# Third tile's Fourier features before the first transposes, VectorE's sums first in each pair, low parts of the up weights a pair ahead

## The reference, cut to what matters

```python
def _attn_ref(q, k, v, lam):          # 2 batches, 8 heads, 768 tokens, 64 wide
    for b in range(nb):               # blocks of 64 tokens
        intra = (qb @ kb.T * Dmask) @ vb
        out[block] = intra + (qb * lam_pow) @ kv_state
        kv_state = lam_block * kv_state + (kb * rev_pow).T @ vb

def _moe_ref(x, w_ch1, w_ch2):        # x is 2 x 768 x 512
    X = np.fft.fft(np.fft.fft(x, axis=1), axis=2)
    u = x + np.real(X)
    un = (u - mean(u)) / sqrt(var(u) + 1e-6)
    return u + np.maximum(un @ w_ch1, 0.0) @ w_ch2      # 512 -> 2048 -> 512

def _moe2_ref(x, g_ln, w_ch1, w_ch2): # the same without the transform, with a gain g_ln
    ...
```

## Time and profile before

| | |
|---|---|
| median of 3 runs | 627.78 us (626.17 to 630.95) |
| the profiled execution | 626.12 us |
| its span, first to last instruction | 624.2 us |
| mean granted TensorE clock | 0.981 |
| busy: TensorE, VectorE, ScalarE, GpSimd | 595.3, 371.4, 242.6, 151.9 us |

### The profile page before, as it was taken

The page is one execution under the profiler, slowest core; times in us unless marked ns, Lnnn a source line. Parts: engine busy times, 40 slices in busy tenths (PEclk is TensorE's granted clock), DMA queues, the critical chain, the costliest instruction groups (busy, mean ns, idle before and its releaser), DMA issues.

```text
span 624.2 us, 10828 instructions
## 1 busy us (share of the span) xinstructions
PE 595.3 (95%) x4124; PEld 409.2 (66%) x4124; DVE 371.4 (60%) x637; ACT 242.6 (39%) x488; POOL 151.9 (24%) x133
## 2 busy tenths in 40 slices
PE   6999799978989999999999999999999999999997
PEld 3999656745666666666666666576666666666664
DVE  2468967968678586556676898733345334433223
ACT  0223133653465432443356675234422344232231
POOL 1536664643532000110322763001000010000000
PEclk8699799989999999999999999999999999999999
DMA  7999790000000253231122231100001000010001
GB/s 227 330 372 390 275 316 9 1 2 0 1 2 1 71 166 103 102 101 43 60 68 86 85 119 51 35 2 1 1 28 42 1 2 0 1 68 1 1 2 68
DMA packets 41412, 50.43 MB, mean 81 GB/s; under 512 B 2442, under 2 KB 28690, under 8 KB 39956
## 3 DMA queue, kind: packets, MB, share of 16 engines
q1 hardware_dynamic: 39156, 45.05, 22.0%
q10 hardware_dynamic: 1728, 3.15, 1.3%
q0 software_dynamic: 480, 1.57, 0.9%
HBM read 43.46 MB, written 6.30 MB: 80 GB/s over the span
## 4 chain that ended last, share of the span: by engine, by line
PE 70%; DVE 13%; issue 7%; POOL 5%; ACT 3%; DMA 2%; SPq 0%; DVEq 0%; ACTq 0%; POOLq 0%
PE bank L572 30%; PE bank L552 26%; PE bank L472 4%; PE bank L409 3%; PE bank L404 2%; PE bank L374 2%; DVE arena L1034 1%; DVE arena L1042 1%; DVE arena L1155 1%; DVE arena L1035 1%; PE bank L541 1%; POOL arena L1410 1%; DVE arena L1149 1%; PE bank L387 1%; DVE arena L1163 1%
## 5 line engine op out<-in xcount | busy, mean ns | idle before, releaser
L572 PE MATMUL bank<-arena 128*128 128x512 f16 x1152 | 287.0, 379 | 3.0 <-DVE arena L1163 2.1
L552 PE MATMUL bank<-arena 128*128 128x256 f16 x2016 | 261.4, 274 | 9.7 <-DVE arena L1204 6.7
L552 PEld LDWEIGHTS bank<-arena 128*128 128x128 f16 x2016 | 197.6, 98 | 84.5 <-DVE arena L1204 7.6
L572 PEld LDWEIGHTS bank<-arena 128*128 128x128 f16 x1152 | 112.3, 98 | 89.6 <-DVE arena L1163 2.7
L1155 DVE SCALAR_TENSOR_TENSOR arena<-arena 128x512 f16<-128x512 f32 x96 | 71.4, 744 | 75.7 <-ACT arena L804 75.6
L804 ACT ACTIVATE arena<-arena 128x512 f16<-128x512 f32 x96 | 60.4, 629 | 101.3 <-DVE arena L1204 95.9
L1198 DVE SCALAR_TENSOR_TENSOR arena<-bank,arena 128x256 f32<-128x256 f32 x48 | 20.2, 421 | 70.9 <-PE bank L552 70.9
L1367 POOL TENSOR_TENSOR arena<-arena 128x512 f32<-128x512 f32 x6 | 8.5, 1412 | 150.8 <-ACT arena L775 90.8
L1149 DVE TENSOR_TENSOR arena<-arena 128x512 f16<-128x512 f32 x42 | 36.3, 873 | 12.2 <-ACT arena L788 12.2
L859 ACT ACTIVATE arena<-bank 128x256 f32<-128x256 f32 x48 | 18.4, 383 | 58.4 <-PE bank L552 58.4
L968 DVE TENSOR_REDUCE arena<-arena 128x1 f32<-128x1024 f32 x32 | 38.3, 1208 | 0.0
(11 more groups left out here) (97 smaller groups left out, 553.0 us busy)
## 6 DMA issues: line engine op xcount, KB each, us to landing
arena<-w SPq DMA_DIRECT2D x48, 256.0 KB, 4.5
arena<-w SPq DMA_DIRECT2D x24, 512.0 KB, 3.7
arena<-attn SPq DMA_DIRECT2D x10, 1024.0 KB, 8.3
x_dram<-arena ACTq DMA_DIRECT2D x12, 256.0 KB, 6.3
out<-arena SPq DMA_DIRECT2D x12, 256.0 KB, 2.1
arena<-attn SPq DMA_DIRECT2D x4, 512.0 KB, 4.3
arena<-c SPq DMA_DIRECT2D x1, 1153.5 KB, 11.1
arena<-g SPq DMA_DIRECT2D x1, 514.0 KB, 12.5
```

Source lines behind the costliest of these rows:

```text
L552: last = nc.tensor.matmul(bank_, wst[:, i, wx, w, kt, :], xs[s % 2][:, ux, x, kt, :], start=not started and k == 0, stop=k == 5, skip_grou ...
L572: last = nc.tensor.matmul(ops[t][:], hT[n % 2][:, half, hx, t * P:(t + 1) * P], wdn[:, i, wx, half * DM:(half + 1) * DM], start=first and ...
```

## The change

It moves instructions and adds no work. The sets of instructions on all engines are the same.

- TensorE: `features(2)` runs ahead of the first transposes, right behind `sequence(12)`; `sequence(13)` runs behind them. The last of the four transposes of stage 0 goes to bank 2 in place of bank 4, and so the transposes wait for `y_done` 12, and sequences 14 and 15 for the copies of the transposes (`ev_done` 4).
- ScalarE's prelude: `up_hi(0,1)` ahead of the first `q_rows`, `q_rows(2)` ahead of `turned`, `down_hi(0,0)` earlier, `y_columns(13)` to `(15)` each a step later.
- VectorE's prelude: `walls(1,2)` and `power_of_two(1)` between `combine(0)` and `combine(1)`; `combine(2)` ahead of the `x_lo`, `down_lo(0,0)` between the second and the third of them.
- VectorE's pairs: `up_lo(0, i+2)` in pair i behind the sums z21 and z22 and the first `hidden_lo`; before it was `up_lo(0, i+1)` ahead of the sums. `row_scale` in the third pair of every stage moves behind the sums as well.
- GpSimd: `up_sums(0,1)` ahead of `add_rows(0)`; `add_rows(2)` between `x_sum(0,1)` and `x_sum(0,2)`.

```diff
--- before.py
+++ after.py
@@ -185,7 +185,7 @@
         kvps = [bank[6 + b] for b in range(B)]
         f1_bank = bank[0:3]
         chain, seventh, spare, ops = [bank[0][:, 0:HT], bank[1][:, 0:HT]], bank[2], bank[3], bank[4:8]
-        first_turn = [bank[3], bank[6], bank[7], bank[4]]
+        first_turn = [bank[3], bank[6], bank[7], bank[2]]
 
         pow_dram = nc.dram_tensor("pow_dram", [H, PITCH], F32).ap()
         x_dram = nc.dram_tensor("x_dram", [B * S, DM], F32).ap()
@@ -650,14 +650,16 @@
             spread_back(1, 2)
             middle_row(0)
             features(1)
-            sequence(range(F1_FIRST, 14))
+            sequence(range(F1_FIRST, 13))
+            features(2)
             pe.wait_ge(fix_done, 1)
             pe.wait_ge(wall_done, 2)
+            pe.wait_ge(y_done, 12)
             for k in range(KT):
                 turn(0, k)
+            sequence(range(13, 14))
+            pe.wait_ge(ev_done, NT)
             sequence(range(14, 16))
-            pe.wait_ge(ev_done, NT)
-            features(2)
 
             for n in range(PAIR * STAGES):
                 pair(n)
@@ -871,27 +873,27 @@
             act.wait_ge(x_out[1], 16 * NBLK)
             up_hi(0, 0)
             y_columns(8)
+            up_hi(0, 1)
             q_rows(0)
             q_rows(1)
             for f in range(9, 12):
                 y_columns(f)
             deviation(0)
-            up_hi(0, 1)
             y_columns(12)
-            y_columns(13)
+            q_rows(2)
             for k in range(KT):
                 turned(0, k)
             x_hi(0, 0)
             x_hi(0, 1)
-            y_columns(14)
+            down_hi(0, 0)
+            y_columns(13)
             x_hi(0, 2)
             x_hi(0, 3)
-            y_columns(15)
+            y_columns(14)
             x_hi(0, 4)
             x_hi(0, 5)
-            down_hi(0, 0)
+            y_columns(15)
             x_hi(0, 6)
-            q_rows(2)
             for n in range(PAIR * STAGES):
                 pair(n)
 
@@ -1187,12 +1189,8 @@
                     combine(LATE[n])
                 if n == 2 * PAIR:
                     tops(2, 5)
-                if prep is not None and i == 2:
-                    row_scale(prep)
                 if prep is not None and i >= 5:
                     x_lo(prep, 2 * i - 9)
-                if s == 0 and 1 <= i < SLOTS - 1:
-                    up_lo(0, i + 1)
                 dve.wait_ge(p4_done, n + 1)
                 dve.wait_ge(u2_out, n + 1)
                 nc.vector.scalar_tensor_tensor(z[n % 2][:, 1, 0:HT], seventh[:, 0:HT], H_SCALE, u2, ALU.mult,
@@ -1207,7 +1205,11 @@
                 if s > 0 and i == 0:
                     add_residual(s - 1, 0)
                     add_residual(s - 1, 1)
+                if s == 0 and i < SLOTS - 2:
+                    up_lo(0, i + 2)
                 if prep is not None:
+                    if i == 2:
+                        row_scale(prep)
                     if n > 0 and i == 0:
                         statistics(prep, (0, 1))
                     if n == 1:
@@ -1261,19 +1263,20 @@
             up_lo(0, 0)
             tops(1, 2)
             combine(0)
+            walls(1, 2)
+            power_of_two(1)
             combine(1)
             statistics(0, range(NT))
-            walls(1, 2)
             row_scale(0)
             normalise(0, range(NT))
-            power_of_two(1)
+            up_lo(0, 1)
+            combine(2)
+            x_lo(0, 0)
+            x_lo(0, 1)
+            down_lo(0, 0)
+            for k in range(2, 7):
+                x_lo(0, k)
             out_scale(0)
-            up_lo(0, 1)
-            for k in range(6):
-                x_lo(0, k)
-            down_lo(0, 0)
-            x_lo(0, 6)
-            combine(2)
             dve.wait_ge(osc_done, 1)
             for n in range(PAIR * STAGES):
                 if n == PAIR * GROUPS:
@@ -1410,13 +1413,15 @@
                     last = nc.gpsimd.tensor_tensor(u, u, mirror(DE[j % 2][:, half, :], half), ALU.add)
                 last.then_inc(addA, 1)
 
+            up_sums(0, 1)
             add_rows(0)
             add_rows(1)
-            up_sums(0, 1)
-            for k in range(4):
-                x_sum(0, k)
+            x_sum(0, 0)
+            x_sum(0, 1)
+            add_rows(2)
+            x_sum(0, 2)
+            x_sum(0, 3)
             up_sums(0, 2)
-            add_rows(2)
             add_rows(3)
             up_sums(0, 3)
             add_rows(4)
```

## The result

| | before | changed |
|---|---|---|
| median of 20 runs each | 626.69 us (625.19 to 631.13) | 629.75 us (627.75 to 631.24) |
| profiled execution, span | 626.12, 624.2 us | 629.07, 627.1 us |
| mean granted TensorE clock | 0.981 | 0.977 |
| TensorE busy | 595.3 us | 597.0 us |

The ratio is 1.0043, with a 95% interval of 1.0029 to 1.0056: 3.1 us more by the medians, 2.9 by the spans. That is within the 1% called no change in advance, but with 20 runs of each the interval lies wholly on the slow side.

A forecast was written before the change was run, and what follows sets the result against it. TensorE bounds the steady pairs; only 110 to 200 us and a 0.3 us wait in stage 2 can move the end. 1.85 plus 1.0 gives 2.85 us more, on a 627.8 us median: 630.6 us, range 624 to 634.5.

The forecast's parts named there:

- d(6): First down group of pair 6 on TensorE, forecast at 197.4 us, 1.85 us behind the kernel before.
- 1.0 in stage 2: row_scale behind the sums delays normalise; stage 2's transposes wait 1.3 us instead of 0.3, 1.0 behind; bounds 0 to 2.
- d(1): First down group of pair 1 on TensorE, forecast at 133.25 us, a gain of 2.0, bounds 0.8 to 4.0.
- signs of being right: Included TensorE idle 3 to 5 us ahead of pair 0 and 1 to 2 us before its last product.
- By turns on the ports: Ahead of pair 0, VectorE and GpSimd alternate instruction by instruction on SBUF; pair 0 begins at 122.3 instead of 118.1.
- the second rival: New waits for y_columns(15) and down_lo put TensorE's clock down: 7.1 us more, 634.9 us; chance 0.1.
- d(2): First down group of pair 2, forecast at 146.95 us, 0.15 ahead of before, after late_features wait 2.1 us.
- d(3): First down group of pair 3, forecast at 161.1 us, 0.1 ahead of before, after waiting 2.3 us for down_lo(0,2).
- the 4.7: TensorE's old waits of 2.4, 1.6 and 0.7 us behind pair 0, up to pair 4, all forecast to go.
- d(4): First down group of pair 4, forecast at 176.4 us, 1.6 behind before, after waiting 3.1 us for down_lo(0,3).
- the waits simply go: Rival for pairs 0 to 5: slack keeps the gains, 7.7 us less, 620.1, chance 0.1; half kept, 624.3, chance 0.15.
- The clock as the way to the slow side: Rival: TensorE's clock falls at new waits ahead of pair 0 and behind down_lo; 7.1 us more, 634.9 us, chance 0.1.

The follow-up runs named there:

- the third experiment: Changed kernel with up_lo(0, i+2) moved to the end of its pair, behind down_lo, the second hidden_lo and normalise: 626.28 us, ratio 0.9974 to the kernel before.
- the second experiment: Kernel before with the pairs of the changed kernel, its own prelude untouched: 632.25 us, ratio 1.0076.
- the last: Changed kernel with up_lo(0,4) alone moved, from pair 2 to pair 3 behind combine(5): 630.01 us, ratio 1.0054 to the kernel before.
- the first four experiments: New prelude with old pairs, 624.52 us; old prelude with new pairs, 632.25; changed kernel with up_lo at pair's end, 626.28, or with GpSimd's weight sums earlier, 623.93.
- the fastest kernel: Changed kernel with weight sums and y_columns(15) earlier, row_scale behind the sums only in stage 0, up_lo placed pair by pair: 618.36 us, ratio 0.9865.

## Why the prediction was right, and which steps were not

It forecast 2.85 us more; 2.9 by the spans and 3.1 by the medians came. (The 630.6 us forecast stood on three runs of the kernel before, 627.78; with 20 runs its median is 626.69, and the changed kernel came at 629.75.) Both parts of the sum were right too: 1.85 behind at d(6) (2.4 measured) and 1.0 in stage 2 (0.8 measured, and 0.9 undone by its experiment).

**Pair 0.** The gain was to be 2.0, with d(1) at 133.25; it came at 132.82, a gain of 2.3. The reason given is confirmed: VectorE's last sum releases the last product (forecast to end at 130.5, measured 130.1), and that product runs at full clock. Several steps were off. The wait ahead of it was to be 1.7 us and is 0.52; the stretch ahead of pair 0 was to be 3 to 5 us and is 2.84. Both lie outside what was named as signs of being right. By turns on the ports, `x_sum(0,2)` was to end at 121.0 and pair 0 to begin at 122.3 after 3.9 us; ScalarE's split of its result starts at 120.00 and pair 0 begins at 121.13 after 2.84. I had the two engines taking turns at every instruction, and they lost less than that. And the clock fell at this wait, which the forecast gave to the second rival. Wait and fall together cost 0.8 us at d(1), by the experiment with `y_columns` one place earlier, which took both away: the path over `features(3)`, the copy of Q and `combine(3)` was not in the forecast, which had VectorE bound by its own list alone. How the 0.8 us divide between the wait and the fall was not tried.

**Pairs 1 and 2.** Late_features were to wait 2.1 us and d(2) to come at 146.95: 2.17 and 146.85. For d(3) a wait of 2.3 and 161.1: 2.22 and 161.35. The waits for the sums in these pairs are gone, as said. One count in the forecast does not hold together: it lets the wait of 1.6 us in pair 4 go, among the 4.7, and two items further on keeps 1.2 of it. It belonged to ScalarE's copy behind `up_hi(0,5)` and not to a sum that the change serves earlier.

**The transposes of stage 1** are the step that was wrong. They were to start at 162.65, waiting for nothing new. They started at 163.90, and what they wait for is the second difference of `combine(5)`, which ends at 163.80. I had read their line as waiting for `normalise` and overlooked the second semaphore. Here the semaphore itself costs only the wait of 0.31 us. Of the 1.25 us by which the transposes are late, 0.25 is d(3) and some 0.7 the clock, which was down after d(3) (six matmuls in 1.48 at 162.11). It stayed without effect: the delays went into slack ahead of d(4), where the wait shrank from the 3.1 I forecast to 2.29. d(4) came at 176.40 where 176.4 was forecast, because it is set by VectorE and GpSimd, not by TensorE. That the two agree so closely is partly luck: `up_hi(0,5)` came 0.2 us late, and the `x_sum` beside `up_lo(0,5)` cost 1.0 us instead of 1.35. For the same reason the 1.2 us at the second product of pair 4 did not show: TensorE was itself late. In the third experiment, where `down_lo` is no longer in the way, the same semaphore costs 3.2 us and brings a fall of the clock of 2.9, and there it spoiled the expectation.

**The port.** The forecast needed an `x_sum` that makes `up_lo(0,5)` wait: L1036 takes 2.29 us at 171.92 beside it. `up_hi(0,5)` came at 168.71 for 168.5. The Trainium skill ("SBUF — State Buffer", section Who interferes with whom) has one of the two engines hold the shared ports for its whole instruction. By that rule VectorE starts its work when `x_sum` ends, at 173.13, and ends near 174.4 (an estimate, with the 1.27 us of the short ones); it ended at 174.21, so the trace agrees within 0.2 us. `x_sum`, which started first, kept its own time, 1.36 us.

**Pairs 4 and 5.** 11.2 and 9.8 us were forecast, 11.44 and 10.00 measured: 0.4 of the 0.55 by which d(6) was missed.

**The rivals.** That the waits simply go fails: 4.7 us of waits behind pair 0 went and 7.3 of new ones came (2.2 and 5.1). The clock as the way to the slow side has its mechanism shown: where I had 1.7 us for a fall, it cost 1.6 in the second experiment, 1.5 in the last, and 2.9 in the third, so the price is not a constant. In the changed kernel it falls twice, at 121 and at 161; of the first, with its wait, 0.8 us reach d(1), and the second does not reach d(4). That was luck as much as reasoning: the wait ahead of d(4) is 2.29 us there only because TensorE came late. With 2.87 and a fall as in the second experiment, the time would have been some 631 (an estimate, 1.6 more). The forecast also said that nothing in the trace of the kernel before lies between waits of 1.65 and 4.3 us, though its own count of waits has one of 2.4:

```profile
155.50 0.83 PE L552 MATMUL bank<-arena 128*128 128x256 f16 x6 [2.37 <-DVE arena L1204]
```

Six matmuls took 0.83 us after it: no fall. So there was a case beside which the 3.9, 2.3 and 3.1 us of the forecast could be laid.

**The question behind it**, where the 4.7 us of waits went, is answered by the first four experiments. `up_lo` is 2.15 us of VectorE's work in each pair, and where there is no slack behind it, it delays `down_lo` and through it TensorE. But VectorE had the time: it idled 3.97 us in pair 2 and 2.97 in pair 3 for a chain that begins on GpSimd, and making the weight sums one step earlier gave most of that back. The forecast had this chain (it has `up_hi(0,4)` end at 154.5, `up_hi(0,5)` start at 168.5), but only as a thing given. Removing either one, `up_lo` ahead of `down_lo` or the late weight sums, took most of the waits on `down_lo` away, so both are needed for them. How much each of the four edits of the fastest kernel is worth within it was not tried.

## What to carry to other kernels

When work is moved out of the way of one wait, list everything that now stands behind it, with the slack of each, and all semaphores of each waiting instruction, not only the one that came last in the old profile; the next one in line takes over as soon as the first is moved. Look for the start of the chain on the engine that feeds the late one: here two steps swapped on GpSimd, which is 24% busy over the span, made more of a difference (5.2 us less by the spans) than moving `up_lo` about on VectorE (2.5 us less in one form, 0.9 more in the other). A delay on an engine that will wait later anyway costs nothing, so give each wait a price only after looking at what ends it next.
